# Attention, token mixing and a gated feed-forward layer in one kernel: loads, stores and three hand-offs in another order

## The reference, cut to what matters

```python
# 1. attention with a decaying state, per batch and head
for t in range(S):
    state = alpha[:, :, t, :, None] * state + np.einsum('bhd,bhe->bhde', k[:, :, t], v[:, :, t])
    y[:, :, t] = np.einsum('bhd,bhde->bhe', q[:, :, t], state)
x = attn_out.transpose(0, 2, 1, 3).reshape(B, S, H * D)
# 2. mixing over the tokens
theta = x @ w_theta
zr, zi = x * np.cos(theta), x * np.sin(theta)
u = x + np.einsum('ts,bsd->btd', w_tok_r, zr) + np.einsum('ts,bsd->btd', w_tok_i, zi)
x = u + np.maximum(u @ w_ch, 0.0)
# 3. feed-forward: h = relu(x @ w_in), convolution over 3 tokens, sigmoid gate
return (h * gate @ w_out)
```

## Time and profile before

| | before |
|---|---|
| median of 3 runs | 542.47 us |
| lowest, highest | 542.22, 544.28 us |
| the profiled execution's own time | 542.66 us |
| span from its first to its last instruction | 540.9 us |
| mean granted TensorE clock | 0.991 of full |
| TensorE matmul busy | 530.0 us (98%) |
| VectorE busy | 443.5 us (82%) |
| ScalarE, GpSimd busy | 287.9 us (53%), 78.6 us (15%) |
| chain of work that ended last: TensorE, DMA, VectorE | 94%, 3%, 1% |
| one load of k, q or the store of x, for one head | 144.0 KB (147.5 kB) |
| one load of a decay, for one head | 146.2 KB (149.7 kB) |
| one load of v, for a pair | 288.0 KB (295 kB) |
| three ordinary weight pieces: w_theta, w_tok_r, w_tok_i | 576.0, 384.0, 384.0 KB |

### The profile page before, as it was taken

One profiled execution on the slowest core, in us unless ns is written; L12 is line 12 of the kernel. 1 busy time (PEld: TensorE's weight loads), 2 busy tenths in 40 slices (PEclk: granted clock), 3 DMA queues, 4 the chain that ended last, 5 costly groups with the idle time before them and its releaser, 6 DMA issues.

```text
span 540.9 us, 11717 instructions
## 1 busy us (share of the span) xinstructions
PE 530.0 (98%) x4116; PEld 522.2 (97%) x4116; DVE 443.5 (82%) x797; ACT 287.9 (53%) x609; POOL 78.6 (15%) x71
## 2 busy tenths in 40 slices
PE   6999999999999999999999999999999999999997
PEld 6899898899999999999999999999999999999997
DVE  7899997998987667866696778899898889889874
ACT  4788787865643443443344543546455554545353
POOL 7788887200000000000000000000000000000000
PEclk8799999999999999999999999999999999999999
DMA  8999999444303020301035002202020211201011
GB/s 190 243 281 262 287 271 318 127 148 147 113 1 118 18 66 17 102 29 54 29 107 180 6 10 80 88 2 87 2 87 0 87 39 48 74 13 44 1 45 44
DMA packets 34106, 52.28 MB, mean 97 GB/s; under 512 B 3568, under 2 KB 24048, under 8 KB 34064
## 3 DMA queue, kind: packets, MB, share of 16 engines
q1 hardware_dynamic: 31248, 47.39, 30.0%
q10 hardware_dynamic: 2816, 4.33, 2.5%
HBM read 37.55 MB, written 14.16 MB: 96 GB/s over the span
## 4 chain that ended last, share of the span: by engine, by line
PE 94%; DMA 3%; DVE 1%; POOL 1%; issue 1%; SPq 0%; ACT 0%; POOLq 0%
PE y_bank L1388 28%; PE y_bank L1447 18%; PE x_bank L1434 9%; PE theta_bank L1434 9%; PE theta_bank L1375 7%; PE y_bank L1418 7%; PE weighed L1292 5%; PE x_sum L1257 3%; PE x_sum L1270 3%; PE turned L1279 2%; PE x_bank L1363 1%; DMA x_scratch<-x_rows 1%; DMA k_in<-in_k_rows 1%; DMA x_in<-x_scratch 1%; PE turned L1297 1%; DVE x_t L1104 1%
## 5 line engine op out<-in xcount | busy, mean ns | idle before, releaser
L1447 PE MATMUL y_bank<-first_w,z 128*128 128x384 f32 x576 | 110.0, 336 | 0.2 <-DVE z L1227 0.2
L1447 PEld LDWEIGHTS y_bank<-first_w,z 128*128 128x128 f32 x576 | 100.9, 188 | 0.5 <-DVE z L1227 0.5
L1388 PE MATMUL y_bank<-first_w,z 128*128 128x384 f32 x432 | 77.8, 338 | 0.0
L1388 PE MATMUL y_bank<-rest_w,z 128*128 128x384 f32 x432 | 76.8, 337 | 0.0
L1388 PEld LDWEIGHTS y_bank<-rest_w,z 128*128 128x128 f32 x432 | 74.5, 188 | 0.1
L1388 PEld LDWEIGHTS y_bank<-first_w,z 128*128 128x128 f32 x432 | 74.3, 188 | 0.0
L985 ACT ACTIVATE out_rows<-theta_bank 128x386 f32<-128x386 f32 x32 | 15.8, 494 | 52.9 <-PE theta_bank L1434 52.9
L1207 DVE TENSOR_SCALAR x_rows<-out_rows,taps 128x384 f32<-128x384 f32 x64 | 26.9, 420 | 20.7 <-ACT out_rows L985 20.5
L1375 PE MATMUL theta_bank<-theta_w,x_t 128*128 128x384 f32 x216 | 41.6, 337 | 0.1
L1214 DVE SCALAR_TENSOR_TENSOR z_full<-out_rows,taps,x_rows 128x384 f32<-128x384 f32 x64 | 39.6, 619 | 2.3
L1210 DVE SCALAR_TENSOR_TENSOR x_rows<-out_rows,taps,x_rows 128x384 f32<-128x384 f32 x64 | 39.6, 619 | 2.3
(11 more groups left out here) (127 smaller groups left out, 971.7 us busy)
## 6 DMA issues: line engine op xcount, KB each, us to landing
k_in<-in_k_rows SPq DMA_DIRECT2D x32, 144.0 KB, 5.1
v_in<-in_v_tokens SPq DMA_DIRECT2D x16, 288.0 KB, 5.4
x_scratch<-x_rows SPq DMA_DIRECT2D x32, 144.0 KB, 4.4
x_in<-x_scratch SPq DMA_DIRECT2D x24, 192.0 KB, 2.6
a_in<-in_a_rows SPq DMA_DIRECT2D x30, 146.2 KB, 4.8
q_in<-in_q_rows SPq DMA_DIRECT2D x28, 144.0 KB, 4.7
y<-x_all SPq DMA_DIRECT2D x7, 576.0 KB, 3.2
u_scratch<-u_sum ACTq DMA_DIRECT2D x6, 576.0 KB, 3.4
```

What stands on the lines that cost most here:

```text
L1388: ins = pe.matmul(y_bank[2 * d + half][:, 0:HALF], z[s % 2][part][zp][:, d * P:(d + 1) * P], mixing_w(part, wp, s)[:, half_tokens(half)], ...
L1447: ins = pe.matmul(out_bank[half][t][:, 0:MODEL], g[k % 4][gp][:, t * P:(t + 1) * P], out_w[wp][f], start=f == 0 and i == 0, stop=f == FF_T ...
```

## The change

1. **Opening.** k and q of pair 0 are loaded in halves (`load_first_k`, and the loop on ScalarE), with semaphores of their own for the first half; the order is a, k, a, k by halves. q of pair 1 is loaded by SyncE, behind k and v of pair 1, and no more by ScalarE.
2. **x of pairs 10, 11 and 12** is copied to three tiles of its own (`x_late`, in the place of `channel_w`, which waits for their stores) and stored in mixing's second tile (`store_late`). Its batch number has to be read too, hence `late_batch`; the two one-element operations for the batch numbers now stand behind the state scan (`place`).
3. **Loads ahead of mixing.** theta's weight stands behind q of pair 14, the first two weight pieces around the judge, and the first x tile in front of the second piece. The pieces alternate w_tok_i, w_tok_r and no more w_tok_r, w_tok_i; sine comes in front of the absolute value and cosine to match.
4. **Passage.** `turn` is split: TensorE's transpose keeps the name, VectorE's subtraction is `lower`. The order in `pair_tail` is another. theta's low part moves from GpSimd to VectorE.
5. **Last projection.** In the last batch the last `front` stands one `back_ff` earlier.

```diff
             if i == JUDGED_AT:
                 do.judge()
             do.scan_state(p)
+            if i == JUDGED_AT:
+                do.place()
         for n in compared_in(i):
             do.compare(n)
         if i == JUDGED_AT - 1:
             do.cap(LAST_PAIR)
         if i == LAST_PAIR:
             do.theta_high()
-            do.theta_low()
         if o >= 0:
             for half in range(2):
                 do.bring(o, half)
                 do.keep(o, half)
         do.refill(i)
-        if i == LAST_PAIR - 3:
-            do.refill_theta()
-        if i in (LAST_PAIR - 2, LAST_PAIR - 1):
-            do.refill_piece(i - (LAST_PAIR - 2))
         if i == JUDGED_AT:
+            do.refill_piece(0)
             do.decide()
-            do.load_first()
+            do.load_first(0)
+            do.refill_piece(1)
+            do.load_first(1)
+            do.load_first(2)
         if o >= 0:
             do.store(o)
-        do.turn(0, 0)
         do.inside(o, 0)
...
-        do.low(0)
-        do.hold(0, 0)
         do.waves()
-        do.theta(0, 0)
-        do.high(1)
-        do.halve(0, 1)
+        do.added(p)
         for half in range(2):
             do.bring(o, half)
             do.keep(o, half)
         do.store(o)
-        do.added(p)
+        do.turn(0, 0)
+        do.lower(0, 0)
+        do.theta_low()
+        do.theta(0, 0)
+        do.turn(0, 1)
+        do.scan_state(p)
+        do.low(0)
+        do.hold(0, 0)
+        do.high(1)
+        do.halve(0, 1)
+        do.hold(0, 1)
         do.angle(0, 0)
-        do.scan_state(p)
         do.sines(0, 0)
-        do.low(1)
         do.inside(p, 0)
         do.inside(p, 1)
-        do.turn(0, 1)
+        do.bring(p, 0)
+        do.bring(p, 1)
+        do.lower(0, 1)
         do.product(0, 0)
-        do.bring(p, 0)
+        do.round_z(0, 0)
         do.keep(p, 0)
-        do.hold(0, 1)
...
                 do.load_weight(s)
+                if s == 1:
+                    do.store_late()
             if s == 4 and not last:
...
                 step(lambda b, k: do.fetch(b, k // FF_TILES, MODEL_TILES + 1 - ahead), b, k + LAG + ahead, last)
-            step(do.front, b, k + LAG, last)
+            if not (last and k + LAG == K - 1):
+                step(do.front, b, k + LAG, last)
             step(do.gate, b, k + LAG - 1, last)
             step(do.split, b, k + LAG - 2, last)
+            if last and k + LAG == K - 2:
+                do.front(b, K - 1)
             do.back_ff(b, k)
 
...
 
-    theta_w, channel_w = (ring(x, 2, [P, MODEL_TILES, MODEL], F32R) for x in ("theta_w", "channel_w"))
+    theta_w = ring("theta_w", 2, [P, MODEL_TILES, MODEL], F32R)
+    with ExitStack() as own:
...
-        def refill_theta():
-            sp.dma_start(theta_raw, theta_piece.source).then_inc(theta_got, 16)
-
         def refill(i):
             if 1 <= i and i + 1 < PAIRS:
                 q_done.done(sp, i - 1)
                 rows(q_in, q_rows, got_q, i + 1)
+            if i == LAST_PAIR - 2:
+                sp.dma_start(theta_raw, theta_piece.source).then_inc(theta_got, 16)
...
-        to_batch = []
+        to_batch = {}
 
         def decide():
-            sp.wait_ge(judged, 3)
+            sp.wait_ge(judged, 4)
             by_state.if_out_of_range(sp, in_range, by_state.path_sync(a_rows, k_rows, q_rows, v_rows, x_scratch, x_stored))
-            to_batch.append(sp.value_load(x_batch[0:1, 0:1], min_val=LAST, max_val=BATCH))
-
-        def store(o):
-            x_copied.done(sp, 2 * o + 1)
+            to_batch[LAST] = sp.value_load(x_batch[0:1, 0:1], min_val=LAST, max_val=BATCH)
+
+        def store_rows(o, sem):
             b, first_head = o // PAIRS_PER_BATCH, 2 * (o % PAIRS_PER_BATCH)
-            assert not to_batch or b == LAST
+            assert not to_batch or b in to_batch
             for g in range(2):
                 at = (first_head + g) * HEAD_DIM
-                sp.dma_start(x_scratch[to_batch[0] if to_batch else b, at:at + HEAD_DIM, :], x_rows[o % 2][head(g), :]
-                             ).then_inc(x_stored[o % 2].sem, 16)
+                sp.dma_start(x_scratch[to_batch.get(b, b), at:at + HEAD_DIM, :], rows_of_x(o)[head(g), :]).then_inc(sem, 16)
+
+        def store(o):
+            if o not in KEPT_LATE:
+                x_copied.done(sp, 2 * o + 1)
+                store_rows(o, x_stored[o % 2].sem)
+
+        def store_late():
+            to_batch[LAST - 1] = sp.value_load(late_batch[0:1, 0:1], min_val=LAST - 1, max_val=BATCH + 1)
+            for o in KEPT_LATE:
+                x_copied.done(sp, 2 * o + 1)
+                store_rows(o, late_stored)
 
...
+        def load_first(s):
+            if s == 0:
+                for t in x_stored:
+                    t.done(sp, PAIRS_PER_BATCH // 2 - 1)
+            load_tile(0, s)
...
+        def load_first_a(chunks, sem):
+            sp.dma_start(a_in[0][half_of(0), columns(chunks, SPAN)], a_first[half_of(0), columns(chunks, SPAN)]).then_inc(sem, 16)
+
+        def load_first_k(chunks, sem):
+            for g in range(2):
+                sp.dma_start(k_in[0][loaded_rows(g, 0), columns(chunks, CHUNK)], k_rows[g, :, columns(chunks, CHUNK)]).then_inc(sem, 16)
+
+        load_first_a(AHEAD, first_a_got)
         sp.wait_ge(pads, 1)
-        rows(k_in, k_rows, got_k, 0)
+        load_first_k(AHEAD, first_k_got)
+        load_first_a(BEHIND, got_a[0].sem)
+        load_first_k(BEHIND, got_k[0].sem)
         sp.wait_ge(pads, 3)
         rows(a_in, a_rows, got_a, 1)
         sp.wait_ge(pads, 4)
         rows(k_in, k_rows, got_k, 1)
         load_v(0)
+        sp.wait_ge(pads, 5)
+        rows(q_in, q_rows, got_q, 1)
         sp.wait_ge(later_pads, 1)
         rows(a_in, a_rows, got_a, 2)
         for t in stored:
...
-            for chunks, a_done, k, b_done, q in ((AHEAD, first_after, first_k, first_before, first_q),
-                                                 (BEHIND, after_done.sem, k_done.sem, before_done.sem, q_done.sem)):
+            for chunks, k_got, q_got, a_done, k, b_done, q in (
+                    (AHEAD, first_k_got, first_q_got, first_after, first_k, first_before, first_q),
+                    (BEHIND, got_k[0].sem, got_q[0].sem, after_done.sem, k_done.sem, before_done.sem, q_done.sem)):
                 pool.wait_ge(a_done, 1)
-                got_k[0].done(pool, 0)
+                pool.wait_ge(k_got, 32)
                 pool.tensor_tensor(chunked(k_scaled[0][:, :])[:, chunks, :], chunked(k_in[0][:, :])[:, chunks, :],
                                    packed(after[0][:, :], 2)[:, chunks, :], ALU.mult).then_inc(k, 1)
                 pool.wait_ge(b_done, 1)
-                got_q[0].done(pool, 0)
+                pool.wait_ge(q_got, 32)
                 pool.tensor_tensor(chunked(q_scaled[0][:, :])[:, chunks, :], chunked(q_in[0][:, :])[:, chunks, :],
                                    packed(before[0][:, :], 1)[:, chunks, :], ALU.mult).then_inc(q, 1)
...
-            if half == 0:
-                x_stored[o % 2].done(act, o // 2 - 1)
-            act.activation(x_rows[o % 2][:, half_tokens(half)], x_sum[:, half, 0:HALF], ACT.Copy).then_inc(x_copied.sem, 1)
+            if half == 0 and o not in KEPT_LATE:
+                x_stored[o % 2].done(act, stored_ahead(o))
+            act.activation(rows_of_x(o)[:, half_tokens(half)], x_sum[:, half, 0:HALF], ACT.Copy).then_inc(x_copied.sem, 1)
+            if n == len(pieces) - 1:
+                act.wait_ge(late_stored, 32 * len(KEPT_LATE))
             act.activation(pieces[n].high, raw_of(n), ACT.Copy).then_inc(piece_high.sem, 1)
...
+            act.activation(sine[:, :], angle[:, :], ACT.Sin).then_inc(sined.sem, 1)
             act.activation(cosine[:, :], angle[:, :], ACT.Abs).then_inc(sized.sem, 1)
-            act.activation(sine[:, :], angle[:, :], ACT.Sin).then_inc(sined.sem, 1)
...
         act.wait_ge(pads, 2)
-        first_q(0)
+        for chunks, sem in ((AHEAD, first_q_got), (BEHIND, got_q[0].sem)):
+            cols = columns(chunks, CHUNK)
+            for slot in range(2):
+                act.dma_start(q_in[0][loaded_rows(slot, 0), cols], q_rows[slot, :, cols]).then_inc(sem, 16)
-        act.wait_ge(pads, 5)
-        first_q(1)
...
+
+        def place():
             dve.tensor_scalar(x_batch[:, :], total[:, :], 0.0, float(LAST), ALU.is_gt, ALU.add).then_inc(judged, 1)
+            dve.wait_ge(judged, 3)
+
+            dve.tensor_scalar(late_batch[:, :], x_batch[:, :], 3.0, float(-2 * LAST - 1), ALU.mult, ALU.add).then_inc(judged, 1)
...
-            if isinstance(b, int) and b == 0 and s == 0:
-                dve.wait_ge(theta_low_done, 1)
-                piece_low.done(dve, SPLIT_EARLY - 1)
-            for part, (wave_of, ready) in enumerate(((cosine, cosined), (sine, sined))):
+            for part, (wave_of, ready) in enumerate(((sine, sined), (cosine, cosined))):
                 ready.done(dve, n)
```

(9 more changed lines are left out.)

68 lines of the change are left out of this document (31 added, 37 removed).

## The result

The changed kernel takes 542.3 us (median of 22 runs, 540.48 to 545.77), the kernel before, run beside it, 544.25 us (22 runs, 542.22 to 547.98). The ratio is 0.9959 (95% interval 0.9941 to 0.9977): 2.2 us, 0.4% faster, within the 0.5% that I called no change. The forecast gain of 2.65 us lies in this interval (1.3 to 3.2 us). The forecast time of 540.0 us doesn't hold, and 542.3 lies 0.3 us above my range. The profiled execution took 542.85 us with a span of 541.1, no shorter than before's 540.9. Two single profiles would thus have shown nothing.

What follows compares the result with a forecast made beforehand. VectorE and the DMA engines were taken to bound attention almost equally, with mixing's start deciding the time. Terms 1.4 + 0.95 + 0.15 + 0.15 = 2.65 us off 542.66 gave 540.0 us, range 537.9 to 542.0.

Steps and rivals of the forecast that it cites:

- part 1: Opening: halved k and q loads start pairs earlier, 2.5 us lead at pair 2, 1.4 us lasting (bounds -1.0 and 2.8).
- part 2: End of attention: late x stores put q of pairs 14 and 15 in time; weighing of pair 15 0.95 us earlier.
- part 3: Passage from attention to mixing: reordered tiles save TensorE's gaps, 0.15 us (bounds 0 and 0.7).
- part 4: Last projection: TensorE's wait of 0.16 us at 532.97 goes, 0.15 us (bounds 0 and 0.2).
- my own sign of being wrong: Wrong in the main if mixing starts after 105.5 us or DMA share falls clearly under 1 between 30 and 75 us.
- the hole: DMA engines' rest between 22 and 31 us, 1.35 us in all, which the earlier opening was to fill.
- the cap: Opening: at most 1.35 us of the lead, the DMA engines' rest, can last; beyond it q is late.
- Rival 1: Opening: the DMA engines follow and the whole lead arrives, 3.75 us gain, 538.9 us; chance 0.27.
- rival 2: Opening: yields nothing that lasts, lead lost in late loads, 1.25 us gain, 541.4 us; chance 0.17.
- The bound of 0.3: Low bound of part 2: TensorE's branch on the judge's number ahead of pair 14's weighing eats most of the gain.
- rival 3: Passage: weighing of pair 15 starts no earlier, 1.55 us gain in all, 541.1 us; chance 0.10.
- Rival 4: Opening: half-size packets cost as much as whole ones, 1.15 us slower, 543.8; shown by pair 1 past 11.3 us; chance 0.08.

Runs made afterwards that it cites:

- before_shifted: Kernel before with an unused 4-byte tile behind x_batch, moving x_t, z and later tiles by 32 bytes; 432.20 us from first mixing matmul to last, no ratio given.
- after_again: The changed kernel profiled and timed once more, no edit; ratio 0.9967 to the kernel before.
- stores_in_step: Changed kernel with x of pairs 10 to 12 stored in its own step again, the new load order kept; ratio 0.9955 to the kernel before.
- old_passage: Changed kernel with transposing and theta back ahead of attention's last groups and theta's low part on GpSimd; ratio 0.9960 to the kernel before.
- weights_early: Changed kernel with theta's weight and the first two weight pieces loaded where the kernel before loads them; ratio 0.9950 to the kernel before.
- number_at_end: Changed kernel with late_batch placed behind all other tiles, so no other tile moves; ratio 0.9951 to the kernel before.
- late_spread: Changed kernel with x of pairs 8, 10 and 12 stored late instead of 10, 11 and 12; ratio 0.9945 to the kernel before.
- compare_late: Changed kernel with the step where ScalarE compares two decays moved from step 7 to step 12; ratio 0.9958 to the kernel before.
- best: compare_late with x of pairs 8, 10, 12 stored late, late_batch behind all tiles, an unused 4-byte number ahead of in_w; 539.87 us, ratio 0.9919.
- after_less_v: Changed kernel without the loads of v of pairs 3 to 13; 539.94 us, ratio 0.9909 to the kernel before.
- before_less_v: Kernel before without the loads of v of pairs 3 to 13; 541.74 us, ratio 0.9959 to the kernel before.
- combined: Changed kernel with late_batch behind all tiles, x of pairs 8, 10, 12 stored late, and zero multiplications in TensorE's idle stretches at 11 to 15 us; ratio 0.9972.
- best_again: The kernel of best run once more, no edit; 542.50 us in the profiled execution, ratio 0.9926 to the kernel before.

## Why the prediction was right or wrong

Means of three profiles of the kernel before (before_shifted among them, up to mixing) against eight with the change or one edit of it (changed kernel, after_again, stores_in_step, old_passage, weights_early, number_at_end, late_spread, compare_late):

| term | forecast | measured |
|---|---|---|
| lead at pair 2 | 2.5 | 17.22 - 14.47 = 2.75 |
| lead at pair 3 | - | 23.08 - 21.68 = 1.40 |
| lead at pair 14 | - | 81.79 - 80.27 = 1.52 |
| lead at pair 15 (part 1, less the judge's second number) | 1.4 | 87.46 - 86.80 = 0.66, + 0.3 for the judge = 1.0 |
| pair 15 to its weighing (part 2) | 0.95 | 7.17 - 5.84 = 1.33, - 0.3 = 1.0 |
| weighing to mixing (part 3) | 0.15 | 12.69 - 12.77 = -0.08 |
| the end (part 4) | 0.15 | 0.46 |
| layout | - | -0.60 |
| sum | 2.65 | 1.77 by these means; 1.95 by medians, 2.2 by the ratio |

**The base is what put the time out of the range.** The step that failed is the last sentence of the sum: "The median of the runs is 542.47, 0.19 lower, which is inside their spread of 542.22 to 544.28; I keep 540.0." Twenty-two runs have a median of 544.25 us, 1.59 us above the 542.66 that I used. Three runs of a kernel that scatters over 5 us were no measure of its middle, and the profile had the earliest mixing of three. 544.25 less 2.65 would have been 541.6, 0.7 us from the result, and the range moved up by 1.59 us (539.5 to 543.6) would have held it. So of the 2.3 us between 540.0 and 542.3 the base is 1.6 and the gain that I put too high is 0.7, by medians. That the gain comes as near as that is in part luck: the layout (0.6 us), part 1 (0.4) and part 3 (0.2) took away, part 4 gave 0.3 back. The range itself has a slip: 2.8, 1.1 and 0.7 us give 538.1, and only with part 4's 0.2 the 537.9 of its low end. And my own sign of being wrong, mixing later than 105.5 us, came: 106.42 us in the first profile, 104.44 to 106.42 over the eight, 105.41 in the mean.

**Part 1** was right for the opening and only half right for what becomes of the lead. Pairs 1 and 2 came within 0.4 us of the forecast. "If TensorE keeps its full clock, the excess of 7.05 over 5.18 us goes as well; if it falls again in its shorter gaps, about half of it stays": it fell at 15 us, and pair 3 was 1.35 us of the lead short. The three runs with the gaps filled show that the time wasn't lost by the clock alone, since pair 5 started no earlier without its fall (32.48, 32.19 and 33.20 us, where the changed kernel has 31.72, the two of best 33.21 and 32.71). The loads were late already: k of pair 2 came 0.7 to 2.2 us behind its scan in 14 of 15 profiles with the new opening, and 0.1 us in all four with the old one. "Beyond 1.35 us the lead turns into q that is late" did not come so. Of the eight, three have a DMA share of only 0.77 to 0.82 from 20 to 26 us, so the hole is not always filled; that the lead at pair 3 is 1.40 us, near the cap, is luck. And from pair 3 to pair 14 nothing more is lost in the mean (1.52 us at pair 14): late q and decays cost both kernels there, and after_less_v shows that the load on the DMA engines makes them late. The rest goes in pair 14, which takes 5.68 us in the mean before and 6.53 after: 0.3 is the judge, and of the other 0.55 most (0.44) stands in the three of the eight where ScalarE waits 1.46 to 1.60 us for the decay of pair 15. Why it does so in these and not in the others stays open. The term was 1.4 and is 1.0. Rival 1 (the whole lead arrives) falls; rival 2 (1.25 us in all) is not ruled out as the lower end of the interval of the ratio.

**Part 2** was the best-sized term (1.0 against 0.95), with the wrong cause: "With 885 kB, 3.2 us at 275 GB/s, out of their way both are in time". q of pairs 14 and 15 is in time with those stores in the way and without them; weights_early shows that it is theta's weight and the first piece behind q that do it (one profile of each). The bound of 0.3 and rival 3 fall: VectorE sets the pace there (5.77 or 5.78 us in twelve profiles). The judge's two operations cost 0.3 us, not 0.2 (pair 14 takes 6.05 us in after_less_v and 5.75 in before_less_v).

**Part 3**: no gain to be measured, and the forecast of 0.15 is within 0.3 of that. x_in, of which I wrote "it lands sooner, as the queue is empty", landed 1.80 us too late in one of two profiles of the changed kernel and 1.03 in the other. In the first it was issued at 90.06 us and ready at 95.06, 5.0 us later, where the kernel before took 4.7 (89.44 to 94.15); the queue wasn't empty, as the first weight piece was issued at 87.78. That theta's low part would be no hindrance was right, and the subtraction took 0.55 us. Rival 4 falls: pair 1 started at 9.14, not past 11.3 us, and while the halves were on their way the DMA engines moved 227 GB/s from 2 to 5 us and 237 from 5 to 8 us, where the kernel before with whole rows has 213 and 224.

**Part 4** was mis-sized threefold, for the wrong row: I took TensorE's wait from the matmul's row (0.16 us), whose start overlaps the modelled end of the one before. The weight load of the same group has it all:

```profile
532.97 4.63 PEld L1447 LDWEIGHTS y_bank<-first_w,z 128*128 128x128 f32 x27 [0.48 <-DVE z L1227]
```

0.48 us, and the end came 0.46 us sooner in number_at_end (431.58 - 431.12), where no tile has moved.

**The layout** was in no term and no rival: "a stretch that this change can shorten by no more than that 0.16 us" is false: mixing got 1.05 us longer, the feed-forward 0.45 us shorter by the layout and another 0.46 by part 4.

## What to carry to other kernels

Where transfers and an engine bound a stage almost equally, count the bytes first: an earlier start is worth only what no load behind it is late for, so look at the loads of the next two pairs before a lead is booked. Take the base from many runs, and before reading one profile's landmarks learn how far a second one moves them. When a new variable is declared, look at what it moves: put it behind all other tiles.

## What the runs showed of the hardware that I had not expected

- Moving tiles by 32 bytes changes TensorE's pace with no wait in the trace: mixing tiles 8.13 to 8.25 and 8.16 us with x_t and z moved, feed-forward steps 3.1600 to 3.1534 us with in_w and what lies behind it moved (best). It isn't the address by itself: the last tiles of batch 0 ran at 8.13 us in old_passage, after_less_v and before_shifted with x_t and z moved, and at 8.25 in the changed kernel. Why stays open.
- TensorE stopped for 1.02 to 1.32 us amid a group (until 72.07 us in the changed kernel, 23.02 in combined, 66.45 in best_again), in other places each time, in 3 of 19 profiles and in neither of the two with less load on the DMA engines, which is too few to tie it to that load. That it waited for its own instructions, which also come by DMA (the page's queue named instruction, 0.43 MB), would fit; it wasn't tried.
- The DMA share of 1.00 doesn't say whether loads are late. In best it is 1.02 from 26 to 80 us with every pair in step:

```profile
26.00:80.00 54.00, 53.74 (x1020) 50.73 (x1018) 51.28 (x53) 45.12 (x95) 45.54 (x32) 1.00 1.02 278
```
